# Three straddling tiles as plain fp32 products, copies shared between VectorE and ScalarE, and the w_out2 split moved on GpSimd in a packed-attention and feed-forward kernel

## The reference

```python
def sm_attn(qq, kk, vv):              # softmax(q k^T / 8) v
    ...
p_packed = sm_attn(p, k, v)           # 32 rows per head
x = sm_attn(q, p_packed, p_packed)    # 576 rows per head, 32 keys
...                                   # x becomes (4608, 512)
h = x @ w_in                          # 512 -> 1024
solu = h * softmax(h)
ln = (solu - mean) / sqrt(var + 1e-6) * g_ln
x = ln @ w_out                        # 1024 -> 512
h = max(x @ w1, x @ w2, x @ w3)       # 512 -> 768
out = h @ w_out2                      # 768 -> 512
```

## Time and profile before

| | |
|---|---|
| median of 3 runs | 1035.26 us (1034.15 to 1037.35) |
| the profiled execution, its own time | 1035.78 us |
| its span, first to last instruction | 1034.0 us |
| TensorE busy | 1001.0 us, 97% |
| VectorE, ScalarE, POOL busy | 609.7, 348.4, 269.0 us |
| attention ends, first network's last product ends | about 154 us, 488.7 us |

### The profile page before, as it was taken

The page is one execution under the profiler, slowest core; times in us unless marked ns, Lnnn a source line. Parts: engine busy times, 40 slices in busy tenths (PEclk is TensorE's granted clock), DMA queues, the critical chain, the costliest instruction groups (busy, mean ns, idle before and its releaser), DMA issues.

```text
span 1034.0 us, 14973 instructions
## 1 busy us (share of the span) xinstructions
PE 1001.0 (97%) x6050; PEld 806.9 (78%) x6050; DVE 609.7 (59%) x984; ACT 348.4 (34%) x559; POOL 269.0 (26%) x228
## 2 busy tenths in 40 slices
PE   7997789999999999999999999999999999999998
PEld 5655458788888888887888888888888888888887
DVE  2888889856665678556466636656355725553021
ACT  4766544433433424324122332214122331223111
POOL 0368652957947585600000000000000000000000
PEclk9999999999999999999999999999999999999999
DMA  8988734346443363215754435543546345442351
GB/s 283 387 276 293 260 129 169 102 165 219 171 165 144 140 231 123 82 63 208 289 210 165 185 121 195 214 170 126 182 184 214 146 159 182 175 153 92 112 163 41
DMA packets 47269, 183.17 MB, mean 177 GB/s; under 512 B 8160, under 2 KB 8160, under 8 KB 37600
## 3 DMA queue, kind: packets, MB, share of 16 engines
q1 hardware_dynamic: 40976, 147.21, 40.2%
q0 software_dynamic: 6224, 35.00, 8.9%
HBM read 134.62 MB, written 47.58 MB: 176 GB/s over the span
## 4 chain that ended last, share of the span: by engine, by line
PE 81%; DVE 11%; ACT 4%; issue 3%; POOL 1%; DMA 0%; ACTq 0%; DVEq 0%
PE ps L1133 28%; PE ps L766 26%; PE ps L1165 14%; PE ps L1156 5%; PE ps L1035 2%; PE ps L875 1%; ACT a L1237 1%; DVE h_lo L1525 1%; DVE spot L1847 1%; DVE bn L1714 1%; DVE packedT L1585 1%; PE ps L780 1%; DVE spot L1838 1%; DVE a2T L1620 1%; POOL a L668 1%
## 5 line engine op out<-in xcount | busy, mean ns | idle before, releaser
L1133 PE MATMUL ps<-ys,slot 128*128 128x512 f32 x1512 | 346.1, 390 | 0.6
L1133 PEld LDWEIGHTS ps<-ys,slot 128*128 128x128 f32 x1512 | 283.2, 188 | 62.8 <-ACT spot L1208 3.9
L1838 DVE TENSOR_TENSOR spot<-ps,spot 128x512 f32<-128x512 f32 x108 | 74.3, 688 | 104.6 <-PE ps L1133 75.4
L1208 ACT ACTIVATE spot<-ps 128x512 f32<-128x512 f32 x90 | 52.8, 596 | 208.1 <-PE ps L1133 197.1
L766 PE MATMUL ps<-ln_lo,w_out_s_hi 128*128 128x512 f32 x280 | 109.0, 389 | 0.0
L766 PE MATMUL ps<-ln_hi,w_out_s_lo 128*128 128x512 f32 x280 | 109.0, 389 | 0.0
L766 PE MATMUL ps<-ln_hi,w_out_s_hi 128*128 128x512 f32 x280 | 108.9, 389 | 0.0
L1165 PE MATMUL ps<-w_out_s_lo,h_hi 128*128 128x512 f32 x216 | 84.0, 389 | 0.0
L1165 PE MATMUL ps<-w_out_s_hi,h_hi 128*128 128x512 f32 x216 | 84.0, 389 | 0.0
L1165 PE MATMUL ps<-w_out_s_hi,h_lo 128*128 128x512 f32 x216 | 84.0, 389 | 0.0
L1341 ACT ACTIVATE u<-ps,neg_max 128x1024 f32<-128x1024 f32 x36 | 40.2, 1118 | 126.0 <-DVE neg_max L1696 126.0
(11 more groups left out here) (158 smaller groups left out, 1488.5 us busy)
## 6 DMA issues: line engine op xcount, KB each, us to landing
slot<-w_operands SPq DMA_DIRECT2D x36, 1792.0 KB, 7.2
w_operands<-stage POOLq DMA_DIRECT2D x18, 1024.0 KB, 4.9
v_raw<-in_v_dram SPq DMA_DIRECT2D x8, 1152.0 KB, 6.3
q_raw<-in_q_dram SPq DMA_DIRECT2D x32, 288.0 KB, 5.1
y_features<-yst SPq DMA_DIRECT2D x9, 1024.0 KB, 4.4
y_raw<-y_features SPq DMA_DIRECT2D x9, 1024.0 KB, 5.3
out_dram<-spot SPq DMA_DIRECT2D x36, 256.0 KB, 2.1
slot<-w_operands SPq DMA_DIRECT2D x9, 1024.0 KB, 5.1
```

Source lines behind the costliest of these rows:

```text
L1133: last = pe.matmul(ps[:, group_bank(g, k), :], w[:, a - 1, i, kk, :], ys[:, b, j, kk, :], start=n < 4 and kk == 0 and e == 0, stop=kk == K ...
L1208: return act.activation(dst, src, ACT.Copy)
L1838: dve.tensor_tensor(dst[:, :], a, b, op).then_inc(ready, 1)
```

## The change

On SP and in the memory plan, tiles 13, 22 and 31 get operands of their own in plain float32. They lie in the space of w_out2's split parts, and SP loads them from HBM in its single queue. SP's `load_slot(0)` gets one more wait.

```diff
+    straddle_m = place_at(cursor[0] - 2 * K2 * DM * 4, "straddle_m", [P, 2, QUADS, FF1])
+    straddle_a = place_at(cursor[0] - 2 * K2 * DM * 4 + 2 * QUADS * FF1 * 4, "straddle_a", [P, 2, QUADS, TAIL])
...
+            def load_straddle(q):
+                if q > 1:
+                    sp.wait_ge(h_filled, 9 * (q - 1) + 5)
+                for x in range(2):
+                    at = slice(S - TAIL, S) if x == 0 else slice(0, TAIL)
+                    sp.dma_start(straddle_m[:, x, :, :], m_dram[2 * q + x]).then_inc(straddle_loaded, 16)
+                    sp.dma_start(straddle_a[:, x, :, :], a_dram[2 * q + x][:, :, at]).then_inc(straddle_loaded, 16)
...
                     load_y(0, 0)
+                    sp.wait_ge(a_stored, 16 * (B - 2))
+                    load_straddle(1)
+                elif t in (3, 5):
+                    load_straddle((t + 1) // 2)
...
             sp.wait_ge(w_stored[1], 16 * GROUPS)
+            sp.wait_ge(w_out2_split, K2 // 2)
             load_slot(0)
```

```diff
+            def load_w_out2(n):
+                dst = weight_raw[n % 2][:, :].rearrange("p (k n) -> p k n", k=2)
+                pool.dma_start(dst, w_out2_v[:, 2 * n:2 * n + 2, :]).then_inc(w_out2_loaded[n % 2], 16)
+            def split_w_out2(n):
+                hi, low = (w[:, 2 * n:2 * n + 2, :] for w in w_out2_s)
+                raw = weight_raw[n % 2][:, :].rearrange("p (k n) -> p k n", k=2)
+                wait_alone(pool, w_out2_loaded[n % 2], 16 * (n // 2 + 1))
+                pool.tensor_scalar(hi, raw, 1.0, None, ALU.mult).then_inc(w_out2_hi, 1)
+                wait_alone(pool, w_out2_hi, n + 1)
+                pool.tensor_tensor(low, raw, hi.bitcast(F32), ALU.subtract).then_inc(w_out2_split, 1)
...
-            lo_w_out(B - MEAN_STEP - 3)
+            hi_w_out(K1 // 2 - 1)
+            lo_w_out(K1 // 2 - 1)
...
-                load_piece(n)
+                load_operands(n)
             block_scale(0)
-            wait_alone(pool, a_stored, 16 * (B - 2))
-            wait_alone(pool, m_stored, 16 * (B - 2))
-            wait_alone(pool, t_filled, 1)
-            for n in range(W2_END):
-                split_piece(n)
             s = 0
             for t in range(1, BLOCKS):
                 block_scale(t)
                 for _ in range((0, 1, 2, 1, 1, 2, 1, 1, 0)[t]):
                     split_operands(s)
                     s += 1
+            for n in range(2):
+                load_w_out2(n)
+            wait_alone(pool, h_filled, 9 * 3 + 5)
+            for n in range(K2 // 2):
+                split_w_out2(n)
+                if n + 2 < K2 // 2:
+                    wait_alone(pool, w_out2_split, n + 1)
+                    load_w_out2(n + 2)
```

```diff
+                if n > 9 and len(terms) > 1:
+                    for g in range(QUADS):
+                        for w in range(WIDE):
+                            for x in range(2):
+                                last = pe.matmul(ps[half(x), bank + w, :], straddle_a[:, x, g, :],
+                                                 straddle_m[:, x, g, w * 512:(w + 1) * 512],
+                                                 start=g == 0, stop=g == QUADS - 1)
+                    last.then_inc(h_filled, 1)
+                    return
...
                     up(0, 0)
+                if b == MEAN_STEP + 1:
+                    column_means()
                 if first:
                     turn_k(b + 2, 2)
+                if b == MEAN_STEP + 1:
+                    scores2(b, 1)
+                if first:
                     turn_k(b + 2, 3)
-                if b == MEAN_STEP:
-                    column_sums()
-                if b == MEAN_STEP + 1:
-                    column_means()
+                if third and first and b != MEAN_STEP + 1:
+                    scores2(b, 1)
                 if second:
                     turn_a1(b + 1)
-                if third:
+                if third and not first:
                     scores2(b, 1)
                 if first:
...
-                    pe.wait_ge(t_hi, TPB * t + TPB)
-                    for w in w_out_s:
+                    for part in range(2):
+                        at = slice(part * 2 * P, (part + 1) * 2 * P)
+                        pe.wait_ge(t_hi, TPB * t + 2 * part + 2)
+                        for w in w_out_s:
+                            for c in range(K1):
+                                pe.matmul(ps[:, part, 0:2 * P], w[:, c, 0:P], ln[0][:, c, at],
+                                          start=w is w_out_s[0] and c == 0, stop=False)
+                    pe.wait_ge(t_split, TPB * t + TPB)
+                    for part in range(2):
+                        at = slice(part * 2 * P, (part + 1) * 2 * P)
                         for c in range(K1):
-                            pe.matmul(ps[:, y_bank(t, m), :], w[:, c, 0:P], ln[0][:, c, :], start=w is w_out_s[0] and c == 0,
-                                      stop=False)
-                    pe.wait_ge(t_split, TPB * t + TPB)
-                    for c in range(K1):
-                        last = pe.matmul(ps[:, y_bank(t, m), :], w_out_s[0][:, c, 0:P], ln[1][:, c, :], start=False,
-                                         stop=c == K1 - 1)
+                            last = pe.matmul(ps[:, part, 0:2 * P], w_out_s[0][:, c, 0:P], ln[1][:, c, at], start=False,
+                                             stop=c == K1 - 1)
```

On ScalarE, all three copies of `a1T` and half of `packedT`'s; `copy_columns` goes to the end of step 2:

```diff
+            def copy_packedT(b):
+                act.wait_ge(packedT_filled, b + 1)
+                src = turned("packed", b)[:, 0:QUADS * P].rearrange("c (y l n) -> c l y n", l=2, n=NPACK)
+                dst = packedT[b % 2][:, :, :].rearrange("c (y l) n -> c l y n", l=2)
+                for jj in range(2):
+                    last = copy(dst[half(jj), 1], src[half(1), 1])
+                last.then_inc(packedT_second, 1)
...
                     exp1(b + 1, 1)
+                if b == MEAN_STEP + 1:
+                    copy_mean()
                 if first:
                     copy_k(b + 2, 2)
                     copy_k(b + 2, 3)
                 if second:
-                    copy_a1(b + 1, 0)
-                    copy_a1(b + 1, 2)
-                if b == MEAN_STEP:
-                    copy_columns()
-                if b == MEAN_STEP + 1:
-                    copy_mean()
+                    for part in range(3):
+                        copy_a1(b + 1, part)
                 if third and not first:
                     exp_h(0, 0)
-                if first:
-                    copy_k(b + 2, QH)
                 if third:
                     exp2(b, 0)
                 if first:
+                    copy_k(b + 2, QH)
...
                     exp2(b, 1)
                 if second:
+                    copy_packedT(b + 1)
                     copy_q(b + 1, 2)
```

On VectorE, those copies are gone, and `centre` takes one row block at a time:

```diff
-                for l in range(2):
-                    for jj in range(2):
-                        last = dve.tensor_copy(dst[half(jj), l], src[half(l), l])
+                for jj in range(2):
+                    last = dve.tensor_copy(dst[half(jj), 0], src[half(0), 0])
...
                     max2(b, 0)
-                if second:
-                    copy_a1(b + 1)
                 if third and not first:
                     max_h(0, 0)
                 if third:
                     turn_in(b, 1)
                     max2(b, 1)
                 if MEAN_STEP < b < B - 2:
-                    centre(b - MEAN_STEP - 1)
+                    centre(b - MEAN_STEP - 1, 2 * (b - MEAN_STEP - 1))
                 if third and not first:
                     solu(0, 0)
                 if third:
...
                 if second:
                     take_packed(b + 1)
                 if third and not first:
-                    centre(b - MEAN_STEP - 1)
                     max_h(0, 1)
                 if second:
                     copy_packedT(b + 1)
...
                     turn_out(b, 0)
                 if second and not first:
                     copy_q(b + 1, QH)
+                if MEAN_STEP < b < B - 2:
+                    centre(b - MEAN_STEP - 1, 2 * (b - MEAN_STEP - 1) + 1)
                 if third:
...
                 max2(b, 1)
+                centre(K1 // 2 - 1, K1 - 2, K1 - 1)
                 inverse2(b, 0)
```

More of the change, by code:

```diff
@@ L293, in raw_count @@
     def raw_count(n):
-        return sum(16 if c < W2_END else 32 for c in range(n % 2, n + 1, 2))
+        return 32 * (n // 2 + 1)
     def rows(t):
@@ L391, in y_bank @@
     def y_bank(t, m):
-        return 0 if t == BLOCKS - 1 and m == 0 else 6 + m % 2
+        return 6 + m % 2
     def merged_of(b):
```

79 lines of the change are left out of this document (37 added, 42 removed).

## The result

The changed kernel takes 1043.91 us (median, 1042.13 to 1044.56 over 5 runs), the kernel before 1035.26 (1034.15 to 1037.35). The ratio is 1.0075, 95% interval 1.0062 to 1.0089: slower by 8.7 us. The profiled execution has a span of 1042.3 us where before had 1034.0.

The account below looks back on a forecast made before the run. TensorE, busy 1001.0 of 1034.0 us, was taken as the bound, with VectorE setting the pace in attention. 1034.0 - 7.5 - 6.0 + 12.7 + 9.8 = 1043.0 span, 1044.3 median; 8-in-10 range 1035 to 1053.

Parts of the forecast that it names:

- Attention and block 1: Attention steps and block 1: copies moved to ScalarE, POOL no longer splitting w_out2 near 190; 7.5 us less.
- the prediction's 1.0, 1.8 and 3.6: Attention steps: running gain in us expected up to steps 0, 3 and 5.
- The bound of 10.1: Attention: at most 10.1 us from VectorE losing 1.26 us of copies in each of eight steps.
- Three plain tiles: Tiles 13, 22 and 31 as plain products: 3.5 us each, 2.0 less per tile, 6 us less.
- The rival in which the halves run in turn: Straddling tiles: the two halves run one after the other, 3 x 3.5 us more, 1055; chance 8%.
- Tile 13: Ahead of tile 13: TensorE waits 11.0 us for straddle operands queued behind y's read-back, plus 1.7 of clock; 12.7 more.
- Group 0: Ahead of group 0: slot and y's second half wait for POOL's w_out2 splits; 8.1 late plus 1.7 clock, 9.8 more.
- the clock's 1.7: Behind each of the two waits: TensorE at granted clock 0.50 for a while, charged 1.7 us.
- POOL's chain: Ahead of group 0: POOL's w_out2 loads and three splits from 461.55, ready at 484.3, then slot 0 and y's half.
- What costs nothing: down(8, 0) in halves (up to 1.3 us if uncovered), the last w_out pair, tiles 22 and 31: no effect.
- A faster attention of 16 us: Steps -1 to 6: VectorE bounds attention throughout, all 16 us comes off, median 1026; chance 9%.
- One wait mostly covered: One of the two waits mostly covered, such as group 0 only 0 to 3 us late; about 1037, chance 13%.

Follow-up runs that it names:

- e10: Attention of the kernel before put back into e4, all else of e4 kept; 1026.31 us, ratio 0.9905.
- e8: Kernel before with only the attention part of the change, w_out2 split where it was before; 1029.48 us, ratio 0.9941.
- e6: e4 with the eight products of a straddle tile ordered strip by strip instead of alternating; 1026.44 us, ratio 0.9910.
- e3: Changed kernel with tile 13's straddle operands loaded ahead of the store of y of block 0; 1031.10 us, ratio 0.9954.
- e12: Changed kernel with ScalarE's copies of y of the last block's first two down projections ahead of its first y split; 1045.96 us, ratio 1.0093.
- e5: e4 with down(8, 0) whole again, after all four tiles are transposed and copied; 1023.37 us, ratio 0.9879.
- e1: Changed kernel with w_out2's loads and splits moved on POOL ahead of block_scale(8); 1034.84 us, ratio 0.9990.
- e4: Changed kernel with both moves: w_out2 ahead of block_scale(8), straddle operands ahead of the store of y of block 0; 1021.04 us, ratio 0.9859.
- e2: Changed kernel with tile 13 in three passes from resident operands again, its straddle load dropped; 1032.73 us, ratio 0.9970.

## Why the prediction was right, and where its sizes were off

The forecast was 1044.3, the result 1043.91. The mechanism held, two transfers that come too late in their queues against three gains. That the number fits to 0.4 us is partly luck: the tiles saved about 1.0 less than forecast and group 0 lost 2.1 less. Term by term:

**Attention and block 1, -7.5.** Measured 7.2, by the store of y of block 1. The two halves hold: 5.5 from the steps (5.3 to 6.0 in e10 and e8) and 2.1 from POOL's leaving block 1 (1.9). Inside the steps the forecast is right by errors that cancel. POOL's second scaling of a step starts 1.04 us earlier than before in step 0, 0.63 in step 1, 0.07 later in step 2, and then 0.75, 2.24, 4.13 and 6.36 earlier in steps 3 to 6; the prediction's 1.0, 1.8 and 3.6 up to steps 0, 3 and 5 stand beside 1.04, 0.75 and 4.13. Steps 1 to 3 lost 0.3 where 0.8 was forecast as gain, steps 4 and 5 won 3.4 where 1.8 was. By the store of y of block 0 the 6.36 have shrunk to 5.3, which was not followed further. What the prediction read too kindly is the new order: the wait for VectorE's turn_in, which it named, is 2.2 us in step 1, with a slower clock behind it in most profiles. In e7, without it, the same scaling starts at 37.37, 52.52 and 68.85 in steps 0 to 2 (before 39.10, 54.40, 72.05). The bound of 10.1 from VectorE's own saving was rightly not taken.

**Three plain tiles, -6.0.** 3 x (5.45 - 3.58) = 5.6, less about 0.2 a tile at its two ends: 5.0. The column sums were the right row for it: eight products in 3.5 predicted, 3.58 measured. The 0.2 is what the sum had put at nothing. Ahead of tile 22 the last product of the stream has 0.31 us and behind tiles 13 and 31 the next one 0.33 or 0.34, where the stream has 0.227. The Trainium skill (TensorEngine Tiling (Array Packing), Key Properties) says that a change of tiling mode drains TensorE. The trace agrees in so far as a gap of about 0.1 us stands at either end, somewhat less than the 0.16 that the prediction estimated. That the mode makes it, and not the change from fp32r to plain fp32, is not shown. The rival in which the halves run in turn was false, and its price of 3.5 a tile too: e6 gives 1.8.

**Tile 13, +12.7.** 10.1 of wait and 2.7 of clock make 12.8, and e3 gets back 12.8. Wait and clock were each off by about a microsecond, in opposite directions. The transfers landed at 245.6, where the prediction, moved by the 7.2 us that the stretch ahead was shorter, has 253.5 - 7.2 = 246.3. The clock took 2.7 where I charged 1.7: it stayed at 0.50 nearly to the end of the tile, whose 3.65 us became 6.35.

**Group 0, +9.8.** 7.7 in place of 8.1, and the clock's 1.7 did not move group 0. This is the term that was mis-sized. Each link is as predicted to within a microsecond (loads landed at 466.6, splits to 484.6, y's half 9.3 after its issue, group 0 at 497.2 for 496.8). The prediction named POOL's chain alone as what sets the time; VectorE's slowed split of y reached the same point at the same moment, and it was not foreseen. I also let TensorE wait in one piece. In fact VectorE's split of y ran beside POOL's splits and slowed, ScalarE's copies of y queued behind it, and the wait broke into 5.3 and 1.5 with 12.9 us of products between. The clock fell behind the 5.3, and its 2.0 us were hidden in group 0's wait. e12 has the wait in one piece: 9.1, a clock of 0.50 behind it with nothing left to hide it, and 2 us more.

**What costs nothing.** The two parts of down(8, 0) were hidden by the wait for group 0, as said; uncovered they are worth 1.25 (e5) for the 1.3 predicted. The last w_out pair cost nothing that shows. Tiles 22 and 31 did not wait.

**The sum.** -7.2 - 5.0 + 12.8 + 7.7 = +8.3, and 8.3 lie between the spans. From the end of tile 13 to the last block's transposes it is 3.2 us shorter, where the two tiles in it save 3.3 by these figures (3.7 without their ends).

**The rivals.** A faster attention of 16 us was far off. "One wait mostly covered" was not so; its price was given as about 1037, where the prediction's own terms make 1034.5 to 1037.5 of it. The medians of e1 (1034.8) and e3 (1031.1) are what it would have been with the one or the other covered in full.

The best version by its median is e7, though not clear of e4: the changed kernel with w_out2 split ahead of block_scale(8), the straddle operands loaded ahead of the store of y of block 0, and the second scores back behind turn_a1. It takes 1019.69 us, ratio 0.9840 (0.9824 to 0.9856), 16 us below before and 24 below the change as it was made.

## What to carry to other kernels

A saving on a full engine is only as good as the arrival of its operands: before an edit is costed by what the engine saves (5.6 us here), put the new transfer's issue time, from the queue it stands in, beside the time at which the engine arrives (here the last transfer went out 1.3 us after TensorE was ready, and took 8.8 to land). Work moved off one contended stretch must be put into an idle one; POOL had 20 idle us right ahead of the place chosen, and using them was worth 9.1 us. A wait in the list is a cost only if removing it moves what comes next; e12 removed 5.3 us and won nothing.

## What was unexpected about the hardware

**VectorE beside POOL.** The second subtraction of the y split, with two inputs in SBUF, took 2.77 us while POOL split w_out2 and 0.69 when it did not. VectorE in time, changed kernel near 470, and then e1:

```profile
470.00 2.77 DVE L1862 TENSOR_TENSOR turn<-y_raw,turn 128x512 f32<-128x512 f32 x1
472.70 2.77 DVE L1577 TENSOR_TENSOR ys<-y_raw,ys 128x1024 fp32r<-128x1024 f32 x1
...
480.81 0.68 DVE L1872 TENSOR_TENSOR turn<-y_raw 128x512 f32<-128x512 f32 x1
```

```profile
469.81 0.69 DVE L1863 TENSOR_TENSOR turn<-y_raw,turn 128x512 f32<-128x512 f32 x1
470.42 1.22 DVE L1578 TENSOR_TENSOR ys<-y_raw,ys 128x1024 fp32r<-128x1024 f32 x1
```

That is a factor of 4 and of 2.3, more than the 1.7 of the m_even row; I had seen that row and not applied it to y's split. The first of them begins at 470.00, inside POOL's subtraction from 469.47 to 472.23, and ends 0.5 us behind it. The Trainium skill (SBUF — State Buffer, Who interferes with whom) says that a VectorE instruction with two inputs in SBUF contends with a GpSimd instruction that reads SBUF. For these rows the trace agrees. It is not always VectorE that pays: the subtraction at 480.81 has two inputs in SBUF as well and took its 0.68, inside a POOL split that took 3.21 us (from 478.86) where the other two took 2.79. A list of such pairs ahead of group 0 would have shown VectorE's split and ScalarE's copies late.

**The clock behind a wait.** Behind the 10.1 us of wait it was 0.50 over the stretch from 246 to 249, behind e12's 9.1 over 494 to 502. Behind the 5.3 us it was 0.50 from 482 to 486 and 0.93 from 486 to 490. Around the 2.2 us wait in step 1 it fell in eight profiles of ten; the same code then has POOL's scaling in step 2 at 72.12 (the changed kernel) or 70.77 (e4), 1.35 us apart. In e2, e6 and e8 the 2.2 us wait came about 1.1 to 1.4 us earlier, and they reach 70.7 to 71.0 at 0.76.

**Strips side by side.** Two strips of 64 columns of plain fp32 products overlap fully if their products alternate (0.43 us for one record of each), and for about four of the sixteen records even when they are issued one strip after the other.
